# Delta-rule attention and two expert layers on one core: feature moves in 6 transfers on two queues, features padded to 128 rows, the order around the first inverse, and a turn of 12 slots for VectorE

## The reference, cut to what matters

```python
def _attn_ref(q, k, v, beta):                      # 4 x 8 heads, 768 steps, 48 features
    k_n = k / (norm(k) + 1e-06)
    for t in range(S):
        y[:, :, t] = einsum('bhd,bhde->bhe', q[:, :, t], state)
        v_old = einsum('bhde,bhd->bhe', state, kt)
        state = state + bt * einsum('bhd,bhe->bhde', kt, vt - v_old)

def _moe_ref(x, domain_probs, w1, w2):             # 3072 rows, 384 features, 4 experts, F = 1024
    p = domain_probs / (domain_probs.sum(-1, keepdims=True) + 1e-09)
    for e in range(E):
        out += p[:, e:e + 1] * (maximum(x @ w1[e], 0.0) @ w2[e])

def _moe2_ref(x, expert_emb, tau, w1, w2):         # 8 experts, each row goes to its best one
    logits = normalized(x) @ normalized(expert_emb).T / tau
    expert_idx = argmax(logits, axis=1)
    for e in range(E):
        out[mask] = gate_w[mask, None] * (maximum(x[mask] @ w1[e], 0.0) @ w2[e])

reference = _moe2_ref(_moe_ref(_attn_ref(q, k, v, beta)))
```

## Time and profile before

| | |
|---|---|
| median of 3 runs | 1482.67 us (1478.38 to 1484.53) |
| the profiled execution's own time | 1468.24 us |
| its span | 1466.5 us |
| its mean granted TensorE clock | 0.946 |
| TensorE busy | 1333.5 us, 91% of the span |
| VectorE, ScalarE, GpSimd busy | 640.5, 470.8, 632.9 us |

### The profile page before, as it was taken

How to read it: one execution, slowest core, us unless ns; L and a number is a source line. 1 busy time by engine, 2 the same in 40 slices (tenths; PEclk the granted TensorE clock), 3 DMA queues, 4 the chain that set the end, 5 groups by cost and what they waited for, 6 DMA issues and landing times. The chain is left out here.

```text
span 1466.5 us, 32008 instructions
## 1 busy us (share of the span) xinstructions
PE 1333.5 (91%) x13279; PEld 1156.4 (79%) x13280; DVE 640.5 (44%) x1048; ACT 470.8 (32%) x794; POOL 632.9 (43%) x660
## 2 busy tenths in 40 slices
PE   4469999899997999989998999999899299999996
PEld 4457888688886888778887888888777299999996
DVE  6833545426443364434643344232642244535342
ACT  2213323253233432333322433334433133424231
POOL 4181337633485236842469323554453222222221
PEclk7579999999999999989999999999999599999998
DMA  8034223533435234262342333336333133334310
GB/s 199 2 104 119 74 88 105 133 100 67 103 114 131 83 68 115 83 158 84 60 120 76 94 89 69 107 103 201 92 94 129 33 119 124 119 133 138 123 30 22
DMA packets 68321, 146.77 MB, mean 100 GB/s; under 512 B 13172, under 2 KB 28977, under 8 KB 67048
## 3 DMA queue, kind: packets, MB, share of 16 engines
q1 hardware_dynamic: 56296, 114.70, 28.8%
q10 hardware_dynamic: 6912, 18.88, 3.9%
q0 software_dynamic: 4992, 11.44, 2.6%
HBM read 132.71 MB, written 11.48 MB: 98 GB/s over the span
## 5 line engine op out<-in xcount | busy, mean ns | idle before, releaser
L426 POOL TENSOR_TENSOR wsl<-raw,wsh 128x768 fp32r<-128x768 f32 x146 | 267.9, 1837 | 469.2 <-ACT wsh L542 468.9
L778 DVE SCALAR_TENSOR_TENSOR hl<-bank,hh 128x512 fp32r<-128x512 f32 x192 | 132.5, 690 | 549.3 <-ACT hh L546 542.8
L546 ACT ACTIVATE hh<-bank 128x512 fp32r<-128x512 f32 x192 | 114.7, 598 | 629.5 <-PE bank L1170 629.5
L1168 PE MATMUL bank<-xhl,wsh 128*128 128x512 f32 x576 | 229.9, 399 | 39.8 <-POOL wsl L426 24.5
L1181 PE MATMUL bank<-hh,wsh 128*128 128x512 f32 x576 | 236.2, 410 | 1.4 <-DVE tmp L808 1.4
L1169 PE MATMUL bank<-xhl,wsh 128*128 128x512 f32 x576 | 228.3, 396 | 0.0
L1170 PE MATMUL bank<-xhl,wsl 128*128 128x512 f32 x576 | 228.3, 396 | 0.0
L1182 PE MATMUL bank<-hh,wsl 128*128 128x512 f32 x576 | 227.7, 395 | 0.0
L1183 PE MATMUL bank<-hl,wsh 128*128 128x512 f32 x576 | 226.7, 394 | 0.0
L542 ACT ACTIVATE wsh<-raw 128x768 fp32r<-128x768 f32 x192 | 160.7, 838 | 11.1 <-DMA raw<-in_w_soft 11.0
L1168 PEld LDWEIGHTS bank<-xhl,wsh 128*128 128x128 f32 x576 | 110.8, 192 | 66.4 <-POOL wsl L426 27.0
(11 more groups left out here) (206 smaller groups left out, 2149.3 us busy)
## 6 DMA issues: line engine op xcount, KB each, us to landing
raw<-in_w_soft SPq DMA_DIRECT2D x192, 384.0 KB, 3.2
rawT<-in_w_top ACTq DMA_DIRECT2D x48, 384.0 KB, 3.6
kq<-in_kq SPq DMA_DIRECT2D x24, 384.0 KB, 11.3
pb<-p_scratch SPq DMA_DIRECT2D x24, 256.0 KB, 4.0
rawT<-in_w_top SPq DMA_DIRECT2D x16, 384.0 KB, 6.2
kN<-in_kn SPq DMA_DIRECT2D x6, 768.0 KB, 7.0
vN<-in_vn SPq DMA_DIRECT2D x6, 768.0 KB, 5.3
xs_scratch<-xrow SPq DMA_DIRECT2D x20, 192.0 KB, 3.7
```

The lines of the kernel that those rows point to most:

```text
L426: nc.gpsimd.tensor_tensor(wsl[:, n % WB, :], raw[:, n % RB, :], f32(wsh[:, n % WB, :]), ALU.subtract).then_inc(wlp_ok, 1)
L546: nc.scalar.activation(hh[:, n % 2, :], ps_h[n % 2][:, :], ACT.Relu).then_inc(hi_ok, 1)
L778: nc.vector.scalar_tensor_tensor(out=hl[:, n % 2, :], in0=ps_h[n % 2][:, :], scalar=0.0, in1=f32(hh[:, n % 2, :]), op0=ALU.max, op1=ALU.su ...
L1168: nc.tensor.matmul(o, wsh[:, w, cols], x_hi, start=(kk == 0), stop=False)
```

## The change

Four edits.

- `move_x` is issued by two engines: SyncE moves the rows of the first head of a pair, ScalarE those of the second, three transfers each, each with the high and the low part together (16x2x512), for all tokens at once, in piece 0 too.
- `kq` has 128 rows in memory too (16 rows of zeros after each 48), and one transfer brings it instead of two. The loads at the start are in another order: kN(0), beta, kq(0, k), kq(0, q), vN(0), kq(1, k).
- The two memsets of the inverse are a function of their own, `start_inverse`; VectorE does those of piece 0 first of all. GpSimd masks the scores, waits for VectorE's inverse to end, and then does the values of piece 0 and the two low weights.
- `inverting` has 12 slots where it had 10.

```diff
-    X_MOVES = 2 * 2 * KM
+    X_MOVES = 2 * KM
...
     def inverting(m):
         begun = [SPT * t + INV_SLOT + LATE[t] for t in range(NT - 2)]
-        return m < 6 or any(b <= m < b + 10 for b in begun)
+        return m < 6 or any(b <= m < b + 12 for b in begun)
...
+    def move_features(eng, c, hh2):
+        for k in range(KM):
+            src, dst = (f32(xhl[rows, c % 2, :, kk, :]) for rows, kk in (
+                (slice(HALF * hh2 + 16 * k, HALF * hh2 + 16 * k + 16), KM),
+                (slice(HALF * hh2 + D, HALF * hh2 + HALF), k)))
+            eng.dma_start(dst, src).then_inc(x_mv, 16)
...
-            for hh2 in range(2):
-                sp.dma_start(kq[ROWS_D[hh2], c % 2, i, :, :, :].rearrange("p a c n -> p (a c n)"),
-                             kq_d[c, hh2, :, i]).then_inc((k_in, q_in)[i][c % 2], 16)
+            sp.dma_start(kq[:, c % 2, i, :, :, :].rearrange("p a c n -> p (a c n)"),
+                         kq_d[c, i]).then_inc((k_in, q_in)[i][c % 2], 16)
...
-        load_features(0, 0)
         load_kn(0)
         sp.dma_start(beta[:, :, :], beta_d).then_inc(b_in, 16)
+        load_features(0, 0)
+        load_features(0, 1)
         load_v(0)
-        load_features(0, 1)
...
         constants()
+        mask_scores()
+        pool.wait_ge(inv_step, INV_STEPS)
         values(0)
-        mask_scores()
         for n in range(2):
             low(n)
+        start_inverse(pool, nc.gpsimd, 1)
         invert(pool, nc.gpsimd, 1)
...
+            if a == 19 and c < NC:
+                move_x(c)
...
         for b in (bank[6], bank[7], bank[2], bank[3]):
             nc.vector.memset(b[:, :], 0.0).then_inc(ps_zero, 1)
+        start_inverse(dve, nc.vector, 0)
         embeddings()
```

More of the change, by code:

```diff
@@ L29, in program @@
 def program(nc, keep, kq_d, kn_d, vn_d, beta_d, probs_d, w_soft, w_top, emb, tau, out, p_d, xs, table):
-    NC, _, D, _, _ = kq_d.shape
+    NC = kq_d.shape[0]
+    D = kn_d.shape[3]
     E1, NF, _, WCOLS = w_soft.shape
@@ L231, in x_of_half, with start_inverse @@
         return cols.rearrange("p k (b c n) -> p b k c n", c=NCH, n=HALF)[:, :, :, ch, :]
[L233 to L236, removed]
+    def start_inverse(eng, ops, c):
+        flat = Tblk[:, :, :].rearrange("p i j -> p (i j)")
         if c:
@@ L239, in invert @@
         ops.memset(flat, 0.0).then_inc(inv_step, 1)
-        eng.wait_ge(inv_step, first + 1)
+        eng.wait_ge(inv_step, INV_STEPS * c + 1)
         ops.memset(flat[:, 0:BLK * BLK:BLK + 1], 1.0).then_inc(inv_step, 1)
+    def invert(eng, ops, c):
+        T = Tblk
+        first = INV_STEPS * c
         eng.wait_ge(inv_step, first + 2)
@@ L295, in load_p, with move_x @@
                              pb_in[i % 2], 16)
[L297 to L312, removed]
+        def move_x(c):
+            sp.wait_ge(xl_ok, UN * (c + 1))
+            move_features(sp, c, 0)
         def store_rows(t, j):
@@ L338, in sync @@
         sp.dma_start(table.rearrange("(p r) c -> p r c", p=P), fill[:, :, :]).then_inc(fill_out, 16)
-        for half in range(NCH):
-            move_x(0, half)
+        move_x(0)
         sp.wait_ge(p_set, 1)
@@ L359, in sync @@
                 load_v(t + 2)
-            if a == 19 and 0 < t + 1 < NC:
+            if a == 19 and t + 1 < NC:
                 move_x(t + 1)
@@ L464, in gpsimd @@
                 values(t + 2)
+                start_inverse(pool, nc.gpsimd, t + 2)
                 invert(pool, nc.gpsimd, t + 2)
@@ L536, in x_high, with move_x @@
             nc.scalar.activation(xhl[LIVE, c % 2, 0, :, cols], ps_yT[LIVE, :, :], ACT.Copy).then_inc(xh_ok, 1)
+        def move_x(c):
+            act.wait_ge(xl_ok, UN * (c + 1))
+            move_features(act, c, 1)
         def w_high(n):
@@ L985, in gram @@
             if v == 0:
-                pe.wait_ge(k_in[c % 2], 32 * (c // 2 + 1))
+                pe.wait_ge(k_in[c % 2], 16 * (c // 2 + 1))
                 if c >= 2:
@@ L1036, in scores @@
             if v == 0:
-                pe.wait_ge(q_in[c % 2], 32 * (c // 2 + 1))
+                pe.wait_ge(q_in[c % 2], 16 * (c // 2 + 1))
                 if c:
@@ L1159, in up @@
                 pe.wait_ge(xl_ok, UN * (t + 1))
-                pe.wait_ge(x_mv, 16 * X_MOVES * (t + 2))
+                pe.wait_ge(x_mv, 16 * X_MOVES * (t + 1))
             pe.wait_ge(*low_done(n))
@@ L1539, in features @@
     def features(a):
-        return a.reshape(B, H // 2, 2, NC, 2, HALF, D).transpose(3, 2, 6, 0, 1, 4, 5).reshape(
+        a = a.reshape(B, H // 2, 2, NC, 2, HALF, D).transpose(3, 2, 6, 0, 1, 4, 5).reshape(
             NC, 2, D, B * H // 2, 2, HALF)
+        return np.pad(a, ((0, 0), (0, 0), (0, HALF - D), (0, 0), (0, 0), (0, 0)))
     def tokens(a):
@@ L1557 @@
     arrays = {
-        "kq": np.ascontiguousarray(np.stack([features(k)[..., late_first], features(q)], axis=3)).reshape(
-            NC, 2, D, 2, -1),
+        "kq": np.ascontiguousarray(np.stack([features(k)[..., late_first], features(q)], axis=1)).reshape(
+            NC, 2, P, -1),
         "kn": tokens(k), "vn": tokens(v),
```

## The result

| | before | after |
|---|---|---|
| median of 4 runs on the same chip | 1483.6 us (1478.38 to 1487.06) | 1419.53 us (1416.41 to 1420.58) |
| ratio after / before, 95% interval | | 0.9567 [0.9535, 0.9600] |
| the profiled execution, its span | 1468.24, 1466.5 us | 1416.41, 1414.6 us |
| mean granted TensorE clock | 0.946 | 0.969 |
| TensorE busy | 1333.5 us, 91% | 1315.2 us, 93% |

The change makes the kernel 4.3% faster. The forecast was 1437 and the range ended at 1421: the direction was right, the size was not. The two profiled executions lie 51.8 us apart, where the sum of the prediction was 45.6; the medians lie 64.1 apart, and a repeat of the comparison gave 56.5.

The account below looks back on a forecast made before the run. The prediction took the kernel as a chain up to TensorE's first slot, then a row of slots of 18 matmuls each unless a wait comes in. Terms 7.1 + 7.3 + 3.6 + 27.6 = 45.6; 1482.67 - 45.6 = 1437 us, range 1421 to 1454.

Parts of the forecast that it names:

- The turns: VectorE's turn in tiles 0 to 3: 12 slots end TensorE's waits for GpSimd's low weights, 27.6 us gained (20 to 29).
- the first rival: In VectorE's turn, the wait moves to the fourteenth slot, costing 12 us in three tiles: 1449; chance 0.13.
- The wait that tile 0 was to get instead: At tile 0's border, TensorE waits about 4 us for VectorE's drain, so only 2.1 us are gained there.
- The start up to the end of the first inverse: From kernel start through VectorE's first inverse: memsets 1.1, low weights 3.0, loads 3.0, together 7.1 us gained (1 to 10).
- The second rival: At the start, kq comes later behind kN and the issue wait stays, so nothing shortens: 1445; chance 0.14.
- The moves: Piece 0, last low part to first slot: three issues per queue make 12.1 us into 4.8, 7.3 gained (5.5 to 8).
- The burst behind the first slot: Loads in slots 0 to 2: shorter with 128-row features, fewer low-weight waits and slow matmuls, 3.6 us gained (0 to 5).
- less 1.0: Burst behind the first slot: 1.0 us deducted because TensorE starts a microsecond sooner relative to SyncE's loads.
- The padding: Features in the slots: padding adds 0.5 MB per piece to queues a third busy, costed at nothing.
- The padding's two terms: 128-row features: 3.0 us gained at the start and 3.6 in the burst behind the first slot, 6.6 in all.
- I take the difference over: Whole kernel: the 14.4 us between profiled execution and median of before is carried over to the kernel after.
- The third rival: More than forecast: sooner scores or a clock staying up, and no issue wait, give 54 us, 1429; chance 0.10.

Follow-up runs that it names:

- e1: The kernel before with 12 slots instead of 10 for VectorE's turn, nothing else changed: 1443.85 us, ratio 0.9831 to the kernel before.
- e6: The changed kernel with features of pieces 2 to 5 by two 48-row transfers again: 1435.72 us, 0.9728 of the kernel before, 20.2 us slower than the changed kernel.
- e5: The whole changed kernel measured once more against the kernel before: 1415.56 us, ratio 0.9607.
- e10: The changed kernel with all six moves issued by SyncE and none by ScalarE: 1417.89 us, ratio 0.9619 to the kernel before.
- e12: The changed kernel, mask behind the wait; in tile 0 expert 2's additions and two low weights on VectorE, attention one slot later: 1404.34 us, 0.9526 of the kernel before.

## Why the prediction was too cautious, point by point

- **The turns: right.** In the change three times 8.5 and 2.2 in tile 0 (8.5 and 2.1 forecast), together 27.7 where 27.6 were forecast. The 26.6 measured alone agree in part by luck, as said at e1. GpSimd's first low weights behind the turn are ready in time in every tile, so the first rival fell. In tile 1, TensorE starts slot 63 at 422.52, and slot 65, the first whose low weights are GpSimd's, 2 x 18 x 0.227 = 8.2 later, at 430.7:

```profile
423.77 3.79 POOL L429 TENSOR_TENSOR acc<-acc,tmp 128x512 f32<-128x512 f32 x3
427.52 1.84 POOL L421 TENSOR_TENSOR wsl<-raw,wsh 128x768 fp32r<-128x768 f32 x1
```

  GpSimd's subtraction ends at 429.4, 1.3 us ahead (1.2 forecast). The wait that tile 0 was to get instead came too, 4.1 us for the drain:

```profile
260.61 0.47 PE L1187 MATMUL bank<-hh,wsh 128*128 128x512 f32 x1 [4.14 <-DVE tmp L813]
```

- **The start up to the end of the first inverse: right in sum and in parts.** 55.89 - 48.83 = 7.1, as forecast; memsets 1.1, low weights 3.0, `system` 21.39 - 18.46 = 2.9. The second rival (the start does not shorten) fell. Between there and the last low part 2.4 us more were gained (29.9 against 27.5 us), which no term had.
- **The moves: right** for the first slot (7.3 forecast, 12.1 - 4.7 = 7.4). Alone, their 7.7 in slot 0 shrank to 1.0 in slot 6, behind the burst of narrow features and its slow clock.
- **The burst behind the first slot: mis-sized, the smaller miss.** 3.6 forecast, net 1.0 in the traces (17.3 to 18.3). The waits for VectorE's low weights did go (3.1 to 0.4), the lead rose to 21.3 in slot 5, and then the wait for the inverse of piece 1 took 3.0 of it. What was wrong in it is "less 1.0": what is late next was taken to be SyncE's loads, and GpSimd's inverse of piece 1 was not set against an earlier slot 5.
- **The padding: the step that failed.** "The padding adds 0.5 MB per piece to queues that are a third busy" put the padding in the slots at nothing, from the mean of the whole span; in the bursts the queues are full. The padding's two terms, 6.6 us, measured 20.7 and 23.6. Against the kernel before, the part in the slots is 3.9 in tile 2 and 3.2 in tile 3; with the other edits in, the 48-row transfers cost 7.3 and 4.7 there and 8.4 in tile 0 (e6). It hangs on a row that was in the same view as the earlier trace rows and was passed over, "L1030 <- issue: 3.5". The prediction argued from the issue wait at the start (5.7) that saturated queues make it, and did not look for the same wait elsewhere. Its reading of that wait was right.
- **The level of the forecast.** The sum was 45.6; the traces differ by 51.8, which is 6.2 more, and the medians by 64.1, which is another 12.3. "I take the difference over" put the 14.4 between one profiled execution and the median on top of both kernels, but the kernel after has only some 3 there (1416.41 and 1419.53). The profiled execution of before, 1468.24, lies 10 us below the lowest of its timed runs, and the medians of that same kernel lay at 1470 to 1476 in the other comparisons. From 1472.1, the before of the repeat, the sum makes 1426.5, and 1415.56 was measured: those 11 us are the padding's 20.7 - 6.6 = 14.1, less 1.4 for the other three parts (1.0 and 0.8 under their terms, 0.4 over) and 1.8 by which the whole falls short of its parts. The stated range also ends 2 us below its own sum, 1429 less 6 being 1423; the measured 1419.53 lies outside either way.

The third rival (more than forecast, by 8 us) is nearest in size, though not in mechanism: it rested on the clock and the issue wait at the start, and the gain that was not forecast came from the bursts in the slots.

## What to carry to other kernels

A mean share of the queues says nothing of a burst: for an edit of a transfer's shape, take the windows in which that transfer runs, and every wait in the list that falls into them, "issue" included. A gain at the start is kept only up to the first thing that another engine finishes in its own time, so follow the lead slot by slot and ask which chain does not start sooner. Where a wait for issue is in the list, set the packets of the instruction queue beside it. Sum a change over the executions that one comparison holds, and put the offset between a profile and a median into the range, not into the sum.

## What the runs showed of the hardware

- In stretches with two transfers of 48 rows the queues moved 164 to 182 GB/s, with one of 128 rows 399 to 422, both at a DMA share of about 1: a third more bytes at over twice the rate.
- While the 48-row transfers ran, TensorE had waits of 1.2 to 2.9 us in the middle of a group of matmuls, always before the same matmul, and they came back when only those transfers did. Each ended 1.3 to 1.5 us after the end of a 16 KB packet on the queue of kind "instruction" (five kernels, two tiles each). With the granted clock at 0.58 behind the longer one, those of the kernel before cost 3.9 and 3.2 us.
- Before the products of piece 1, a wait of 1.55 us was followed by four microseconds at a granted clock of 0.57 (108 to 112 us), and one of 1.25 in the same kernel's repeat (e5) by 0.68 there; one of 0.5 (e10) and one of 1.3 (e12) by none (1.00). So the length of a short wait alone did not tell what the clock did.
- VectorE took 4.60 us for a step of 0.36 beside GpSimd's mask of 4.52 (4.57 for one of 0.37, beside 4.66, before). With the mask moved behind the inverse the blocked work is elsewhere: in that kernel VectorE's small norms took 1.09 and 1.73 us beside GpSimd's two low weights, 0.19 each in the kernel after.

```profile
52.09 1.09 DVE L672 TENSOR_TENSOR rroot<-ssq,rroot 128x32 f32<-128x32 f32 x1
53.21 1.73 DVE L674 TENSOR_TENSOR norm<-root,rroot 128x32 f32<-128x32 f32 x1
```
